# The token layer's first product: one fp32 product in place of three fp32r products of split operands

## The reference

```
attn_out = attention(q, k, v, tau)      # (4, 8, 576, 64); scores below max - tau are dropped
x = attn_out.transpose(0, 2, 1, 3).reshape(4, 576, 512)
# token and channel layer
xt = x.transpose(0, 2, 1)
h  = maximum(xt @ w_tok1, 0) @ w_tok2   # w_tok1 576x256, w_tok2 256x576
u  = x + h.transpose(0, 2, 1)
x  = u + maximum(u @ w_ch1, 0) @ w_ch2  # w_ch1 512x1536, w_ch2 1536x512
# gated layer
h  = maximum(x @ w_in, 0); conv of 3 taps over the sequence; out = (h * sigmoid(conv)) @ w_out
```

## Time and profile before

| | |
|---|---|
| median of 3 runs | 849.59 us (848.68 to 851.25) |
| the profiled execution | 850.66 us, its span 848.9 us |
| PE matmul busy | 824.3 us |
| DVE busy | 422.5 us |
| ACT busy | 412.5 us |
| POOL busy | 265.7 us |
| L1146, the first product | 240 matmuls, in bodies 3, 5, .. 17 |
| POOL L471, `xl` | 29.1 us in 16 instructions |
| POOL L440 and L454 on w_tok1 | 7.4 us in 10 instructions |

### The profile page before, as it was taken

One profiled execution on the slowest core, in us unless ns is written; L12 is line 12 of the kernel. 1 busy time (PEld: TensorE's weight loads), 2 busy tenths in 40 slices (PEclk: granted clock), 3 DMA queues, 4 the chain that ended last, 5 costly groups with the idle time before them and its releaser, 6 DMA issues.

```text
span 848.9 us, 15131 instructions
## 1 busy us (share of the span) xinstructions
PE 824.3 (97%) x5656; PEld 669.5 (79%) x5656; DVE 422.5 (50%) x829; ACT 412.5 (49%) x914; POOL 265.7 (31%) x202
## 2 busy tenths in 40 slices
PE   8999999999999998899999999999999999999998
PEld 4666776767777766788888888888899989898996
DVE  6897878787877774501211211211214819156380
ACT  4887887877878785211211201211114737355461
POOL 0062415142332323470200100120291726428170
PEclk9999999999999999999999999999999999999999
DMA  9311111111111114000000000000320010100101
GB/s 266 111 48 47 48 48 46 46 46 46 46 46 46 50 16 149 1 1 0 1 1 1 0 1 1 1 0 1 128 71 2 1 51 1 45 17 0 49 0 62
DMA packets 20906, 32.70 MB, mean 39 GB/s; under 512 B 4416, under 2 KB 11136, under 8 KB 20864
## 3 DMA queue, kind: packets, MB, share of 16 engines
q1 hardware_dynamic: 20864, 32.13, 11.7%
HBM read 27.41 MB, written 4.72 MB: 38 GB/s over the span
## 4 chain that ended last, share of the span: by engine, by line
PE 84%; DVE 6%; ACT 6%; issue 3%; POOL 0%; ACTq 0%; DVEq 0%; POOLq 0%
PE score L1203 17%; PE score L1318 12%; PE score L999 5%; PE out_t L1218 4%; PE turn_y L1218 4%; PE mixed L1218 4%; PE turn_x L1218 4%; DVE prob L858 4%; PE out_t L1303 4%; PE out_t L1094 4%; PE mixed L1146 3%; PE mixed L1094 3%; PE turn_y L1303 3%; PE mixed L1303 3%; PE turn_x L1303 3%
## 5 line engine op out<-in xcount | busy, mean ns | idle before, releaser
L921 DVE SCALAR_TENSOR_TENSOR h<-score,h 128x512 fp32r<-128x512 f32 (+1 forms) x60 | 38.3, 638 | 243.5 <-ACT h L693 243.5
L693 ACT ACTIVATE h<-score 128x512 fp32r<-128x512 f32 (+1 forms) x60 | 33.3, 555 | 250.5 <-PE score L1203 250.5
L841 DVE TENSOR_SCALAR_CACHE_REDUCE negs<-score,neg_scale 128x576 f32<-128x576 f32 x144 | 112.7, 816 | 58.7 <-PE score L999 34.0
L858 DVE SCALAR_TENSOR_TENSOR prob<-negs,thresh,exps 128x576 f32<-128x576 f32 x144 | 134.2, 964 | 0.3 <-ACT thresh L594 0.3
L591 ACT ACTIVATE exps<-negs,neg_max 128x576 f32<-128x576 f32 x144 | 104.6, 772 | 1.9 <-DVE negs L841 1.5
L999 PE MATMUL score<-qk 64*128 64x288 f32 x512 | 85.5, 434 | 1.6 <-DVE negs L841 1.0
L1203 PE MATMUL score<-uh,w1h 128*128 128x512 f32 (+1 forms) x240 | 86.9, 368 | 0.0
L1203 PE MATMUL score<-uh,w1l 128*128 128x512 f32 (+1 forms) x240 | 86.8, 368 | 0.0
L1203 PE MATMUL score<-ul,w1h 128*128 128x512 f32 (+1 forms) x240 | 86.8, 368 | 0.0
L559 POOL TENSOR_TENSOR zl<-z,zh 128x512 fp32r<-128x512 f32 x32 | 54.2, 1694 | 98.7 <-ACT zh_t L779 98.7
L999 PEld LDWEIGHTS score<-qk 64*128 64x128 f32 x512 | 46.9, 188 | 28.0 <-issue 13.1
(11 more groups left out here) (184 smaller groups left out, 2010.0 us busy)
## 6 DMA issues: line engine op xcount, KB each, us to landing
qk<-in_qk SPq DMA_DIRECT2D x16, 640.0 KB, 3.9
vm<-in_v SPq DMA_DIRECT2D x16, 320.0 KB, 4.2
result<-ostage SPq DMA_DIRECT2D x16, 256.0 KB, 2.1
w1f<-in_moe_w_ch SPq DMA_DIRECT2D x4, 768.0 KB, 10.8
w2f<-in_moe_w_ch SPq DMA_DIRECT2D x4, 768.0 KB, 7.4
wif<-in_moe_w_in SPq DMA_DIRECT2D x1, 2048.0 KB, 7.8
wof<-in_moe_w_out SPq DMA_DIRECT2D x8, 256.0 KB, 2.6
wt2f<-in_moe_w_tok SPq DMA_DIRECT2D x1, 576.0 KB, 9.4
```

The source lines that it names most:

```text
L841: nc.vector.tensor_scalar(negs[:, i, h, :].rearrange("p (c s) -> p c s", c=2), raw_of[h], neg_scale[:, 0:1], None, ALU.mult, ALU.min, accu ...
L858: nc.vector.scalar_tensor_tensor(out=prob[:, i, h * S:(h + 1) * S], in0=negs[:, i, h, :], scalar=thresh[:, i, h:h + 1], in1=exps[i][:, h, ...
L921: nc.vector.scalar_tensor_tensor(out=h3[:, n % RING, 1, 0:w], in0=hidden_banks[n % 4][:, 0:w], scalar=0.0, in1=h3[:, n % RING, 0, 0:w].bit ...
```

## The change

`w_tok1` stays in fp32 in one tile `wt1`, and GpSimd no longer splits it. GpSimd's `copy_x` copies `x32` into `xs` (fp32, 256 columns for two pairs) in place of the two instructions of `split_x`. PE computes each `mix_hidden` with 5 fp32 matmuls in place of 15 fp32r ones. The weight is waited for by its loads. The split of w_tok2 stays.

```
-    x_parts = Region(w1l_at - 2 * size([P, NT, 2 * P]))
-    xh = x_parts.put("xh", [P, NT, 2 * P], F32R)
-    xl = x_parts.put("xl", [P, NT, 2 * P], F32R)
+    x_pairs = Region(w1l_at - size([P, NT, 2 * P]))
+    xs = x_pairs.put("xs", [P, NT, 2 * P])
...
-    wt1h = s1.put("wt1h", [P, NT, DT], F32R)
-    wt1l_at = s1.at
-    wt1l = s1.put("wt1l", [P, NT, DT], F32R)
-    wt1f = nc.alloc_sbuf_tensor_at("wt1f", [P, NT, DT], F32, offset=wt1l_at)
+    wt1 = s1.put("wt1", [P, NT, DT])
...
-            def split_x(at):
+            def copy_x(at):
...
-                copy(xh[:, :, mine], x32[:, :, :]).then_inc(xs_hi, 1)
-                pool.wait_ge(xs_hi, pair + 1)
-                pool.nop(nofuse=True)
-                nc.gpsimd.tensor_tensor(xl[:, :, mine], x32[:, :, :], xh[:, :, mine].bitcast(F32), ALU.subtract) \
-                    .then_inc(x_split, 1)
+                copy(xs[:, :, mine], x32[:, :, :]).then_inc(x_copied, 1)
...
-            pool.wait_ge(set_once, 2)
-            def split_wt(kts):
-
-                pool.wait_ge(s_done, 2 * NT)
-                pool.wait_ge(wt_loaded, 3 * DMA)
-                for kt in kts:
-                    split_weight(wt1h[:, kt, :], wt1l[:, kt, :], wt1f[:, kt, :], wt_split)
...
-                if k == 1:
-                    split_wt(range(NT))
                 if k == 2:
+                    pool.wait_ge(wt_loaded, 3 * DMA)
...
 (mix_hidden)
                     if k == 3:
-                        pe.wait_ge(wt_split, NT + KT)
-                    pe.wait_ge(x_split, g - 1)
+                        pe.wait_ge(wt_loaded, 3 * DMA)
+                        pe.wait_ge(set_once, 2)
+                    pe.wait_ge(x_copied, g - 1)
...
-                n = 0
                 for kt in range(NT):
-                    for wt, x in ((wt1h, xh), (wt1l, xh), (wt1h, xl)):
-                        mm = nc.tensor.matmul(mixed[:, 0:2 * P], wt[:, kt, i * P:(i + 1) * P], x[:, kt, :],
-                                              start=(n == 0), stop=(n == 3 * NT - 1))
-                        n += 1
+                    mm = nc.tensor.matmul(mixed[:, 0:2 * P], wt1[:, kt, i * P:(i + 1) * P], xs[:, kt, :],
+                                          start=(kt == 0), stop=(kt == NT - 1))
...
 (mix_out)
+                    if k == 4:
+                        pe.wait_ge(wt_split, KT)
```

More of the change, by code:

```diff
@@ L92, in build @@
     W1_EARLY = 7
-    x_parts = Region(w1l_at - 2 * size([P, NT, 2 * P]))
-    xh = x_parts.put("xh", [P, NT, 2 * P], F32R)
-    xl = x_parts.put("xl", [P, NT, 2 * P], F32R)
-    assert x_parts.at == w1l_at and w1l_at - 2 * size([P, NT, 2 * P]) >= fixed.at + W1_EARLY * size([P, KM, P])
+    x_pairs = Region(w1l_at - size([P, NT, 2 * P]))
+    xs = x_pairs.put("xs", [P, NT, 2 * P])
+    assert x_pairs.at == w1l_at and w1l_at - size([P, NT, 2 * P]) >= fixed.at + W1_EARLY * size([P, KM, P])
     w2l_at = ch1.at
@@ L241, in build @@
         short_x = sem("short_x")
-        x_split = sem("x_split")
+        x_copied = sem("x_copied")
         xt_done = sem("xt_done")
@@ L373, in load_wt @@
             def load_wt():
-                sp.dma_start(wt1f[:, 0:FULL, :], w_tok1[0:MAIN, :].rearrange("(t p) n -> p t n", p=P)) \
+                sp.dma_start(wt1[:, 0:FULL, :], w_tok1[0:MAIN, :].rearrange("(t p) n -> p t n", p=P)) \
                     .then_inc(wt_loaded, DMA)
-                sp.dma_start(wt1f[0:TAIL, FULL, :], w_tok1[MAIN:S, :]).then_inc(wt_loaded, DMA)
+                sp.dma_start(wt1[0:TAIL, FULL, :], w_tok1[MAIN:S, :]).then_inc(wt_loaded, DMA)
                 sp.dma_start(wt2f[:, :, :], w_tok2.rearrange("(t p) n -> p t n", p=P)).then_inc(wt_loaded, DMA)
@@ L457, in _ @@
             chunk_hi = sem("chunk_hi")
-            xs_hi = sem("xs_hi")
-            def split_x(at):
+            def copy_x(at):
                 pair = at.g - 1
@@ L523, in body @@
                 if at.pv:
-                    split_x(at)
+                    copy_x(at)
                 if at.mix:
                     add_u(g - 3)
-                if k == 1:
-                    split_wt(range(NT))
                 if k == 2:
+                    pool.wait_ge(wt_loaded, 3 * DMA)
                     for kt in range(KT):
@@ L657, in normalise_short @@
                 if k >= 1:
-                    act.wait_ge(x_split, pair)
+                    act.wait_ge(x_copied, pair)
                 for h in range(2):
@@ L828, in _ @@
             nc.vector.memset(x32[TAIL:P, FULL, :], 0.0).then_inc(set_once, 1)
-            nc.vector.memset(wt1f[TAIL:P, FULL, :], 0.0).then_inc(set_once, 1)
+            nc.vector.memset(wt1[TAIL:P, FULL, :], 0.0).then_inc(set_once, 1)
             dve.wait_ge(tau_used, 2)
@@ L877, in normalise @@
                 if k >= 1:
-                    dve.wait_ge(x_split, pair)
+                    dve.wait_ge(x_copied, pair)
                     dve.wait_ge(xt_done, pair)
```

## The result

The changed kernel takes 860.99 us (median of 4 runs, 860.26 to 861.87), the kernel before 849.2 us beside it; the ratio is 1.013 with a 95% interval of 1.0114 to 1.0145. It is slower by 11 to 12 us. The forecast was 850.6 with a range up to 854.8.

What follows compares the result with a forecast made beforehand. PE's own work was taken as the bound, with waits for ACT and DVE's mask in the attention stage. Terms -0.6 + 0.6 + 1.1 + 0 = +1.1, taken as +1.0 on median 849.59, gave 850.6 us, range 847.0 to 854.8.

Steps and rivals of the forecast that it cites:

- It is queued at 209.55, waits for the first mask: Odd bodies 3 to 13: `w1h` lets the first mask pass and holds only the second; period -0.1 us.
- My bounds, -2.4 to +1.2: Range in us for six attention periods of two bodies, around a forecast of -0.6.
- The product: Each `mix_hidden` on PE goes from 1.98 to 2.27 us, +0.29; bounds +0.24 to +0.38.
- the extra 0.09 us behind the first record: Delay behind the first matmul of `mix_hidden` after the transposes; forecast to vanish with fp32, +0.38 each if kept.
- the gap before L1064: PE's 0.27 us wait for ACT in an odd body; forecast to absorb 0.2 to 0.3 of the products' 0.58.
- That a mask meets GpSimd and waits: Attention stage: a DVE mask meeting a GpSimd instruction waits until that ends, finishing about 0.6 us later.
- The end: Bodies 15 and 17: the longer products pass through to the time, +0.6 and +1.1 us.
- a switch of 0.09 us at each end: Body 17: cost of going between fp32r units and the fp32 product, 0.18 of its +0.57 us.
- Bodies 1 and 2: Moved weight splits hold the masks about as `xl` did: 0 us, bounds -0.9 and +0.5.
- A: Rival, chance 0.22: nothing is given back, the products' +5.2 us passes whole; 854.8 us.
- C: Rival, chance 0.05: fp32 product dearer, +0.61 each, 855.2 us; by the skill's pages +0.54 each, 858.3.
- B: Rival, chance 0.13: faster, as the second mask behind `copy_x` is no longer held; sum -3.3 us, 846.3.

Runs made afterwards that it cites:

- e6: Changed kernel, with GpSimd also waiting for its own copy of x to finish before the split of w_ch1: 853.7 us.
- e7: Kernel before, with GpSimd's split of x and following weight splits delayed, in bodies 1, 2 and odd ones to 13, until the next body's second mask: 846.2 us.
- e1: Changed kernel, with GpSimd still making a same-shape subtraction behind the copy of x, after a semaphore wait, into an unread buffer: 856.8 us.
- e3: Changed kernel, with GpSimd's split of w_ch1 in bodies 1 to 13 waiting until the second mask behind the copy of x is done: 849.9 us.
- e4: Kernel before, with GpSimd's copy and subtraction of x in bodies 3 to 13 waiting until the second mask behind the products is done: 846.8 us.
- e2: Kernel before without the subtraction making `xl`; the third product reads `xh` instead, same number of matmuls: 847.1 us.
- e9: Changed kernel, with only body 2's split of w_tok2 waiting until the second mask of the next body is done: 856.1 us.

## Why the prediction was wrong

**What failed is one step: "It is queued at 209.55, waits for the first mask".** I had the mask due at 209.31 and the copy's end at 209.45, and let the mask go first by 0.14 us. In the changed kernel the margin is 0.04 us before the copy's end, and the multiplication went first (214.20). Its sum gave -0.1 us a period, -0.6 for six; measured +1.10 and +6.6. With the order that I had assumed, e6's, the period is 40.13 against my 40.0. My bounds, -2.4 to +1.2, varied the length of the hold and the price of the product, but not the order of two instructions 0.14 us apart, though a second hold was the one thing there that could cost a microsecond. The order itself may well have been right at 0.14 us: no run has that margin, but the mask won at 0.16 (e7) and lost at 0.04 to 0.07. So the step failed by the number that it was fed with.

**Why the margin was smaller.** ScalarE's drain h1f and the copy behind it kept their distance of 1.22 us. DVE's score copies came 0.42 us after h1f's start (212.71 against 212.29), before 0.04: they moved on by 0.38 against it, not by 0.29. That is the product, mis-sized:

**The product.** The term that was too small is the one that I dropped, the extra 0.09 us behind the first record. The ten records and the handover stand as forecast (2.25 us from the first record to the scores, forecast 2.27), but the 0.09 is still there, ahead of the first record: four transposes to the first record take 0.50 us, before 0.41. In the kernel before it is the same 0.09 at the same place, only hidden in a first fp32r record that begins early and is long (0.36 us where the others have 0.28). So it is +0.36 where I took +0.29; my upper bound, with the extra kept, was +0.38. Ten records at 0.216 (2.32 us less the last one's 0.38, in nine gaps) against 15 at 0.12 make 0.36. e1 measures it in a period at +0.53 for two, 0.72 less the gap before L1064, which has indeed closed (212.93 to 212.98). I had said 0.2 to 0.3 for that, and 0.2 it is.

**That a mask meets GpSimd and waits** was right: e3, e4 and e6 show it in both directions, 0.81 us free and 1.6 to 2.1 held. That the amount of GpSimd's work is worth nothing was right as well: e1 adds some and is faster.

**The end** was forecast at +0.6 + 1.1 = +1.7. Without the low clock it is +1.5 (e1 and e3, from the four transposes ahead of the first product of body 15 to the first `project`: 40.76 and 40.77 us against 39.28). In e1 body 15 has +0.72 of it, up to the first product of body 17 (27.14 us against 26.42), twice the 0.36, and body 17 the other +0.76. So the 0.6 was a little small, by the product's size, and the 1.1 too much: I had put a switch of 0.09 us at each end of the fp32 product between fp32r units, and there is none, neither ahead of it (the last four fp32r matmuls ahead start at 355.86, the product at 356.76, 0.225 us for each) nor behind (+0.37 by the second matmul behind it, forecast +0.57).

**Bodies 1 and 2** were put at 0, bounds -0.9 and +0.5; measured together +1.4, of which one more stretch of low clock in body 2 is about 1.6. I had counted the low clock only as something that could come back, -1.65, not as something that could double. PE's first wait there, for which the profile names no releaser, grew from 0.40 to 0.83 us as the split of w_tok2 moved forward.

**The rivals.** A, nothing is given back, had the right sign and 854.8: the mechanism was beyond it, as more was taken than given back. C was wrong: the records cost what the rows said, and the page's pass of 109 ns for 256 columns agrees with them (two passes, 0.218, for a record every 0.216). Its +0.54 a product, from the Trainium skill's "FP8 and Floating Point Precision" and "TensorE: Matmul & The Clock Gate", starts too low, since the fp32r product took 1.79 and not 1.64; measured is 0.36 to 0.37. B named the right place, the masks behind `copy_x`, but looked for the good side only.

What the Trainium skill says in "SBUF — State Buffer" (SBUF: two separate sides) would have pointed at the order: a DVE instruction with two SBUF inputs and a GpSimd instruction that reads SBUF hold their shared port pair for a whole instruction, whichever starts first. The traces agree on the whole instruction: each held mask ends 0.6 us after GpSimd's instruction, and the loser waits until the other is done, GpSimd too (1.54 for 1.04 in e2). On who is first the profile's start times don't say it by themselves: in the changed kernel the mask's record starts 0.01 us ahead of `w1h` (214.19 against 214.20), both while the copy still runs, and the mask lost.

## What to carry to other kernels

Where two engines hold each other up for whole instructions, ask of a change which of them arrives first, and by how much; a forecast margin of 0.14 us, of which the bound of the product alone (+0.38 for +0.29) takes 0.09, is worth two outcomes in the range, not one. Here 0.16 us and more decided for the mask and 0.07 and less against it. Work taken from an engine off the path moves all that is queued behind it forward, here onto the masks that PE waits for: e3 and e6 show that one wait, placed well, is worth more than 16 instructions removed. Place such background work by the semaphore of the work it must not meet (e4, e7), and then the two kinds of product differ by only 0.37 us a period.

## What the runs showed of the hardware

- An fp32 matmul cost 1.14 to 1.2 times what three fp32r ones of 128x128x256 did: with the handovers 0.45 us a contraction tile (2.25 / 5) against 0.40 (1.98 / 5), without them 0.43 (ten records 0.216 apart) against 0.36 (1.79 / 5, body 17). An fp32r matmul took 0.12 us for columns that make 0.107 at 2.4 GHz.
- Going from the transposes to the product and from the product to the scores each costs about 0.09 us, whether the product is fp32r or fp32: in the kernel before the first shows behind the first fp32r record, after it ahead of the first fp32 one. Between fp32r matmuls of 512 columns and the product nothing is lost in either kernel (body 17). So it isn't the change between fp32r and fp32 that costs it; what does stays open.
- The granted clock comes in whole stretches. Of 17 runs of the kernel before, those with a mean clock of 0.999 or 1.00 took 848.3 to 848.7 us, those with 0.997 849.5 to 850.5, those with 0.995 851.2 and 851.6: about 1.5 us for each stretch. In body 2 of the kernels before and after, it fell in a window in which PE was busy 2.88 and 2.46 of 4 us, and in e9, with 3.84 us there, it didn't. But a window like that alone doesn't tell: in e1 PE was busy 2.81 us from 64 to 68, in the changed kernel 2.73 from 44 to 48, and the clock stayed at 1.00 there and in the 4 us that followed.
